# Attention chunks taken in order of position, scores by row halves, and an MLP two steps ahead

## The reference

```python
for t in range(S):                                   # attention, per batch and head
    cur = einsum('bhd,bhe->bhde', u * k_t, v_t)
    y[t] = einsum('bhd,bhde->bhe', r_t, state + cur)
    state = w * state + einsum('bhd,bhe->bhde', k_t, v_t)
h = x @ w_in; g = maximum(0.01 * h, h); z = g @ w_out  # MLP
# layer of experts on the tokens with z @ w_skip > 0:
e = argmax(z @ w_gate); out = z + softmax_e * (relu(z @ w1[e]) @ w2[e])
```

## Time and profile before

| | |
|---|---|
| three runs, us | 821.12 median (819.7 to 823.28) |
| span of the profiled execution, us | 822.9; it lies inside the range of the three runs, and so is taken as its own time |
| instructions | 14108 |
| PE busy | 734.3 us (89%) |
| PE weight loads | 685.2 us (83%) |
| DVE busy | 486.6 us (59%) |
| ACT busy | 262.7 us (32%) |
| POOL busy | 208.0 us (25%) |
| chain that ended last, by engine | PE 67%, DVE 22%, issue 4%, ACT 2% |

### The profile page before, as it was taken

One profiled execution on the slowest core, in us unless ns is written; L12 is line 12 of the kernel. 1 busy time (PEld: TensorE's weight loads), 2 busy tenths in 40 slices (PEclk: granted clock), 3 DMA queues, 4 the chain that ended last, 5 costly groups with the idle time before them and its releaser, 6 DMA issues.

```text
span 822.9 us, 14108 instructions
## 1 busy us (share of the span) xinstructions
PE 734.3 (89%) x4327; PEld 685.2 (83%) x4328; DVE 486.6 (59%) x866; ACT 262.7 (32%) x509; POOL 208.0 (25%) x195
## 2 busy tenths in 40 slices
PE   3679999999999999999999999999991489989893
PEld 2679999899989989988898999999991468979793
DVE  7977664666676376566647756643338734464641
ACT  2212223322422422232242233224323153363650
POOL 5422220222232022222203312200002253233322
PEclk9868999999999999999999999999996589999997
DMA  6543322312211231211222122002007267155400
GB/s 210 173 151 116 95 79 77 107 49 61 76 49 49 78 107 49 77 59 59 58 89 76 49 77 97 11 17 70 1 0 304 76 253 259 45 179 193 174 17 7
DMA packets 29445, 77.59 MB, mean 94 GB/s; under 512 B 5096, under 2 KB 17158, under 8 KB 29392
## 3 DMA queue, kind: packets, MB, share of 16 engines
q1 hardware_dynamic: 25872, 62.87, 23.8%
q10 hardware_dynamic: 1728, 9.44, 3.3%
q0 software_dynamic: 1792, 4.56, 1.7%
HBM read 61.48 MB, written 12.19 MB: 90 GB/s over the span
## 4 chain that ended last, share of the span: by engine, by line
PE 67%; DVE 22%; issue 4%; ACT 2%; DVEq 1%; POOL 1%; ACTq 1%; DMA 1%; POOLq 0%
PE bank L555 22%; PE bank L529 17%; DVE am L956 10%; PE bank L628 6%; PE bank L674 6%; PE bank L456 5%; PE bank L510 3%; DVE g_lo L997 3%; DVE am L948 2%; PE bank L488 2%; PE bank L538 2%; PE bank L484 1%; ACT g_hi L737 1%; DVE h_sb L992 1%; PE bank L655 1%
## 5 line engine op out<-in xcount | busy, mean ns | idle before, releaser
L555 PE MATMUL bank<-wout_hi,g_hi 128*128 128x394 f32 x384 | 133.9, 349 | 11.3 <-DVE g_lo L997 11.2
L529 PE MATMUL bank<-x_hi,win_hi 128*128 128x384 f32 x384 | 138.3, 360 | 0.0
L729 ACT ACTIVATE h_sb<-bank 128x384 f32<-128x384 f32 x128 | 63.0, 492 | 221.3 <-PE bank L529 200.6
L555 PE MATMUL bank<-wout_hi,g_lo 128*128 128x394 f32 x384 | 132.1, 344 | 0.0
L555 PE MATMUL bank<-wout_lo,g_hi 128*128 128x394 f32 x384 | 132.0, 344 | 0.0
L529 PE MATMUL bank<-x_lo,win_hi 128*128 128x384 f32 x384 | 130.1, 339 | 0.0
L529 PE MATMUL bank<-x_hi,win_lo 128*128 128x384 f32 x384 | 130.0, 339 | 0.0
L1305 POOL TENSOR_TENSOR kb<-rkt,w_k 64x512 f32<-64x512 f32 x24 | 31.3, 1306 | 379.5 <-PE bank L456 356.9
L997 DVE TENSOR_TENSOR g_lo<-h_sb,g_hi 128x384 fp32r<-128x384 f32 x128 | 80.6, 630 | 75.6 <-ACT g_hi L737 75.6
L992 DVE TENSOR_TENSOR h_sb<-h_sb,bank 128x384 f32<-128x384 f32 x128 | 70.2, 549 | 87.0 <-ACT h_sb L729 86.3
L956 DVE SCALAR_TENSOR_TENSOR am<-const,diag,am 128x128 f32<-128x128 f32 x192 | 116.8, 667 | 3.4
(11 more groups left out here) (160 smaller groups left out, 1085.2 us busy)
## 6 DMA issues: line engine op xcount, KB each, us to landing
raw<-in_experts SPq DMA_DIRECT2D x32, 768.0 KB, 6.1
rkt<-in_rk_t SPq DMA_DIRECT2D x48, 192.0 KB, 3.3
rkn<-in_rk_nat SPq DMA_DIRECT2D x24, 384.0 KB, 3.9
v<-in_v_nat SPq DMA_DIRECT2D x24, 192.0 KB, 2.5
z_rows<-z_sb SPq DMA_DIRECT2D x24, 192.0 KB, 1.9
out<-z_sb SPq DMA_DIRECT2D x24, 192.0 KB, 2.1
stage<-in_win ACTq DMA_DIRECT2D x4, 768.0 KB, 4.6
stage<-in_wout_t ACTq DMA_DIRECT2D x4, 768.0 KB, 5.9
```

The source lines that it names most:

```text
L529: mm = pe.matmul(h_ps[f % 2][:, 0:GT], a[:, kk, cols], b[par][:, kk, :], start=n == 0, stop=n == 3 * KT - 1)
L555: mm = pe.matmul(z_ps[i][:, 0:ZW], a[f % 2][:, tok], b[:, f, :], start=f == 0 and j == 0, stop=f == FT - 1 and j == 2)
L729: act.activation(h_sb[f % 2][:], h_ps[f % 2][:, 0:GT], ACT.Copy, scale=SLOPE).then_inc(s_h_scaled, 1)
```

## The change

The attention and the MLP are written anew, without a loop. What differs:

- **Order of chunks.** Chunk `n` is now position `n // 4` of batch `n % 4`. Four states are kept (one a batch), the state returns to a batch every fourth chunk, and the last four chunks need no state sums. The first four need no state.
- **Scores by row halves.** `kb` has no zeros: a matmul takes 64 rows, heads 2p from partitions 0 to 63 and heads 2p+1 from 64 to 127, each half into a PSUM bank of its own. All eight follow one another in one step.
- **Mask and diagonal.** ACT writes the diagonal into `am` (eight small copies of `ident`, `set_diag`), and DVE lays the scores over it where the triangle is set: two `copy_predicated` of 512 columns.
- **Outputs.** The four matmuls with the state come first, then the eight with v, where before the two kinds took turns; `state_sums` stands right ahead of them.
- **Who computes.** DVE makes `kb` (one instruction) for all chunks, and `kn` and `ruk` from chunk 6 on; POOL makes `kn` and `ruk` of chunks 0 to 5 only. POOL also copies the gate scores, now from `z_sb`.
- **MLP two steps ahead.** `hidden(step+2)` is issued ahead of `project(step)`, with three buffers of `g`.
- **Where chunks stand.** `scores(n)` at step `BEGIN[n]`, sums and outputs two steps later; steps 0, 4, 8 in group 0, then every fifth.
- **DMAs.** Each chunk's y is moved by itself: ten DMAs a chunk. Inputs have two buffers each. ACT issues three stage loads at once at the start; the other weights are split while group 0 runs.

PE's queue in the middle of the kernel before. Shown is the second half of a chunk: `bank<-rt,state` and `bank<-am,v` are outputs, `bank<-v,kn` is the state sum, and `x_hi,win_hi` begins `hidden`.

The core of the diff (POOL's and DVE's order of the prologue left out):

```diff
-BESIDE = [[(i, x) for x in part] for i in range(CPG) for part in ((0,), (1,), (2,), (3, 4))]
+BEGIN = {CPG + i: 4 * i for i in range(CPG)}
+BEGIN |= {CPG * (G + 1) + i: FT * G - 3 + 5 * i for G in range(1, GROUPS - 1) for i in range(CPG)}
+SPLIT_AT = {BEGIN[n] + (4 if n == 5 else 5): n for n in BEGIN}
+POOLED = 6
+LOADS = [("win", 0), ("win", 1), ("gate", 0), ("wout", 0), ("gate", 1), ("wout", 1),
+         ("win", 2), ("gate", 2), ("wout", 2), ("win", 3), ("gate", 3), ("wout", 3)]
...
+        def place_in(n):
+            return n % B * CPB + n // B
...
         # TensorE
-                for i in range(4):
-                    h = 4 * half + i
-                    mm = pe.matmul(scores_bank(n, half)[:, P * i:P * i + P], kb[:, h // 2, h % 2, :],
-                                   rt[k % 2][:, h // 2, :], start=True, stop=True)
+                for p in range(PAIRS):
+                    for q in range(2):
+                        rows = slice(64 * q, 64 * q + 64)
+                        mm = pe.matmul(scores_in(n)[q][:, P * p:P * p + P], kb[n % 2][rows, p, :],
+                                       rt[n % 2][rows, p, :], start=True, stop=True)
...
+            for step in range(STEPS):
+                n = BEGUN_AT.get(step)
+                if n is not None:
+                    scores(n)
+                n = BEGUN_AT.get(step - 2)
+                if n is not None:
+                    if n < CHUNKS - B:
+                        state_sums(n)
+                    outputs(n)
+                if step + 2 < STEPS:
+                    hidden(step + 2)
+                if step in (2, 6, 10):
+                    gate_products((step + 2) // 4)
+                project(step)
...
         # ScalarE
+            def set_diag(n, heads):
+                for h in heads:
+                    ins = act.activation(am_of(n)[h % 2][:, h // 2, :], ident, ACT.Copy,
+                                         scale=diag[n % 2][:, h:h + 1])
+            def high_x(n):
+                act.wait_ge(s_x_in, 160 * (n - CPG + 1))
+                at = P * (n % CPG)
+                act.activation(x_hi[n // CPG % 2][:, :, at:at + P], x_sb[:],
+                               ACT.Copy).then_inc(s_x_hi_done, 1)
+            for p in range(3):
+                load_stage(p)
...
         # VectorE
-                dve.tensor_tensor(am[half][:], scores_bank(n, half)[:].rearrange("a (h t) -> a h t", h=4),
-                                  spread(before, 1, [P, 4, P]), ALU.mult).then_inc(s_masked, 1)
-                for i in range(4):
-                    h = 4 * half + i
-                    ins = dve.scalar_tensor_tensor(am[half][:, i, :], ident, diag[k % 2][:, h:h + 1],
-                                                   am[half][:, i, :], ALU.mult, ALU.add)
+                for q in range(2):
+                    dve.copy_predicated(am_of(n)[q][:], spread(before.bitcast(U32), 1, [P, PAIRS, P]),
+                                        scores_in(n)[q][:].rearrange("a (p t) -> a p t", p=PAIRS)).then_inc(s_masked, 1)
...
         # SyncE
+            def move_y(n):
+                sp.wait_ge(s_y_out, n + 1)
+                if n > CPG:
+                    sp.wait_ge(s_x_hi_done, n)
+                    sp.wait_ge(s_x_lo_done, n)
+                for dst, src in MOVES:
+                    sp.dma_start(x_sb[dst], y_sb[src]).then_inc(s_x_in, 16)
```

1029 lines of the change are left out of this document (525 added, 504 removed).

## The result

The changed kernel takes 785.14 us (median of 4 runs, 783.89 to 788.43) against 821.71 for the one before (819.7 to 823.28) in the same runs: a ratio of 0.957, 95% interval 0.953 to 0.960. It is faster, by 36.6 us where 58 were forecast. The profiled execution has a span of 782.1 us and a time of its own of 783.89, so a time is some 1.8 us more than a span.

The account below looks back on a forecast made before the run. PE's queue was taken to bound the middle and DVE's queue the prologue. Terms summed to -56.1, with a shared edge -57.9, taking 822.9 to 765.0, or 763 on the runs' scale; range 746 to 786.

Parts of the forecast that it names:

- the case as worked: Whole kernel: all terms come out as summed, about 763 us, with 753 to 775 for itself; chance 0.48.
- the wider range: Whole kernel: 746 to 786 us, taking in the better, long-prologue and row-halves-in-turns outcomes.
- rival A: Scores on TensorE: row halves take turns instead of running at once, giving 782 us; chance 0.13.
- rival D: Moves of y: ten DMAs a chunk through single buffers make ACT and PE wait, up to 828 us; chance 0.03.
- The plan's later start: Behind the MLP: copies of z and POOL's copies come before the plan, which starts 1.3 us later.
- the stall (-11): Middle stretch: PE's wait for DVE, 0.57 us a chunk or 12.0 in all, goes but for 1 us.
- 12.6, 18.8 and 1.8: PE's work beside the MLP: us saved by scores in row halves, by outputs, and by an edge counted twice.
- More than the 12.0 can't come back: Middle stretch: if DVE is late again, the loss is at most the 12.0 us of waiting removed.
- the 0.57 a chunk: Middle of the kernel before: of a chunk's 6.47 us on PE, 5.9 is work and 0.57 is waiting.
- the prologue (-19, measured -11.9): Before the first hidden: independent chunks let it start at 35.9 us instead of 54.88, 19 us saved; bounds 29 and 46.
- Rival B: Prologue: large loads ahead of small ones and locks keep it long, hidden at 46, 773 us; chance 0.14.
- The weights (+4): Group 0: weight splits end some 1.5 us after PE wants them at steps 4, 8 and 12, costing 4 us.

Follow-up runs that it names:

- weights_early: The changed kernel with the splits of wout and win beside group 0 one step earlier on ACT and DVE: 785.4 us, ratio 0.958.
- scores_twice: The changed kernel with all 8 score matmuls of a chunk issued a second time right behind the first 8: 803.95 us, one run.
- mask2_first: The changed kernel with DVE masking chunk 2 ahead of low_turned(0) in the prologue: 780.2 us, ratio 0.951.
- adds_pool_lead_one: The changed kernel with the mask by product and eight adds, MLP one step ahead, and POOL making kn and ruk of every chunk: 869.5 us, ratio 1.055.

## Why the prediction was right or wrong

At 785.1 us the time lies outside the 753 to 775 of the case as worked, and just within the wider range, whose top of 786 was there for rival A. The score records rule A out, so that the range holds the time is luck.

**Right.** What bounds the kernel (PE's queue in the middle, a chain through DVE in the prologue). Row halves run in pairs (scores 1.09 us, 1.0 forecast; rival A out). Outputs at 2.03 a chunk, 1.9 forecast without the edge; sums without change in the middle. The predicated copies at the price of a product, no wait of PE for ACT's diagonal copies, POOL's removal worth nothing. The wait for `g_lo` gone. The order of y's moves harmless: 210 moves with a median issue of 591 ns, and ACT in time (rival D out). The plan's later start: `lmax` began 0.7 us behind the last product before and 1.9 after (618.56 - 617.84 and 578.29 - 576.35), 1.2 against 1.3 forecast.

**Wrong, the stall (-11).** The step said that no DVE instruction beside the MLP's own would be late again, since no step got more than 1.7 us of them. I counted how much work DVE had in a step, and checked it against `low_g` alone. I did not ask of the others, `low_x` and `scale_k`, what stands before them and who waits. `low_x` came 1.34 late five times (6.7 us; 6.3 when moved), and `kb`, made last in its step, 0.27 late at some 17 scores, with two longer waits (4.7 in all when moved). Together 11.0, and the middle's shortfall is 10.4. So the term of -11 came out as nothing: the 11.2 us of waits for `g_lo` went, and 12.9 came up in the same queue, for `x_lo` (6.7) and at the scores (3.3, 1.9 and 1.0). By the ledger idle time rose by 2.8 where 7 less was forecast, which is 9.8 of the 10.4. PE's work fell by 32.6 where the terms give 33.2 (12.6, 18.8 and 1.8), and that they agree so well is luck: outputs saved 4 less, and `hidden` and `project` 3.7 and the gate products 2.4 that no term had. "More than the 12.0 can't come back" was wrong too: with the long mask the middle grew by 21.8 and by 64.3.

A slip beside it: the 0.57 a chunk was PE's time per chunk less its work, and that compared groups with unequal contents. Group 7 holds no first `hidden` of a next group, nine matmuls fewer, so a step alone takes (50.8 + 9 x 0.175) / 16 = 3.27 us and not 3.175, and a chunk left about 5.9, waits included. The amount of waiting that I got, 12.0, was close to the 11.2 that the list of waits gives, by luck. The forecast group of 63.4 was too short for this reason, and because chunks come every 5 steps, 3.2 to a group; with the waits gone a group took 64.2.

**Wrong, the prologue (-19, measured -11.9).** Rival B's cause, the large loads ahead of small ones, was at work with 3.7, though not with its 46. The step that failed is the walk of the queues: I had `rkn` ready at 11, DVE at work on it from 13, and took two handovers of 5 us together. In fact DVE's first sum started at 14.7 and the first scores at 16.6, the turn through `y_rows` and `x_hi` cost DVE 5.7 by itself, with the mask of chunk 2 locked behind it (2.4 us of PE's time). And the outputs of a chunk take PE 3.5 to 3.65 there, at the lower level of its clock. With both orders mended the first `hidden` came at 37.2, beside 35.9 forecast.

**The weights (+4)**: 2.6 measured, with 2.33 of it in one wait, and this wait went when the split stood a step earlier.

## What to carry to other kernels

When a stall behind a long instruction is taken away, go through that engine's whole queue again: for every instruction that another engine waits for, what stands directly before it. The work of a step can fit, and two instructions in the wrong order still cost as much as the stall did. Where idle time before a group repeats with the same length and the profile names no releaser, compare its start with the ends of its operands' makers before calling it a price of the hardware. And two edits that cover the same lateness, a shorter task and a longer lead, have no separate gains: each is worth less while the other stands, 4.0 against 46.5 us and 21.8 against 64.3 here. When one wait leaves the list and the time stays, read the whole list again: in `weights_early` another wait had grown.

## What the runs showed of the hardware

- Two 64-row matmuls in different row halves run at once when they are neighbours in the queue: 0.11 us a pair of records, over 16 pairs (one execution) as over 8. With four matmuls of one half between them they do not (1.61 against 1.09 us for 16 records). One more visit to row halves costs about 0.4 us.
- A predicated copy of 128x512 takes 0.67 to 0.73 us, as a product of that shape; a 128x128 diagonal add 0.27 (eight in 2.19) where POOL is idle.
- The first record of `hidden` lasts 0.66 us in the prologue against 0.42 to 0.44 in the middle, and the 16 records of a chunk's outputs in the prologue last 3.65 in one run and 1.88 in another. Where the column shows it (`scores_twice`, `mask2_first`, the half-paced spells of the middle) the granted clock is 0.50 over the longer of these and 1.00 over the shorter; in the kernel after it reads 1.00 over the same durations, so a pace is safer read from the records.
- `low_g` on DVE (both operands in SBUF) takes 0.56 us alone and took 1.35 and 1.21 while POOL's `ruk` and `kn` ran; `leaky`, with one operand in PSUM, kept its 0.54 between them (290.1 us, `adds_pool_lead_one`).
